# Order of ScalarE's work at two places of a fused attention and MLP kernel: a kv copy between two exponentials, and the parting of a tile ahead of W1's sums

## The reference

```
proj = x @ w_phi;  proj -= max|proj| over the 128 features
phi(x) = concat(exp(proj), exp(-proj))          # for q and for k
kv = phi(k)^T v;   z = sum over s of phi(k)
out = phi(q) kv / (phi(q) z + 1e-6)
```

```
block A:  u = x + Re(FFT over both axes of x);  un = layernorm(u);        u + relu(un @ w1a) @ w2a
block B:  un = layernorm(x) * g;                                          x + relu(un @ w1b) @ w2b
```

## Time and profile before

| | |
|---|---|
| median of 3 runs | 1027.41 us |
| the profiled execution's own time | 1027.07 us |
| its span, first to last instruction | 1025.0 us |
| PE busy | 1012.9 us, 99% |
| DVE, ACT, POOL busy | 64%, 58%, 36% |
| mean granted clock of PE | 0.998 |

### The profile page before, as it was taken

One profiled execution on the slowest core, in us unless ns is written; L12 is line 12 of the kernel. 1 busy time (PEld: TensorE's weight loads), 2 busy tenths in 40 slices (PEclk: granted clock), 3 DMA queues, 4 the chain that ended last, 5 costly groups with the idle time before them and its releaser, 6 DMA issues.

```text
span 1025.0 us, 17118 instructions
## 1 busy us (share of the span) xinstructions
PE 1012.9 (99%) x6028; PEld 936.4 (91%) x6028; DVE 657.5 (64%) x1156; ACT 591.8 (58%) x1036; POOL 368.5 (36%) x364
## 2 busy tenths in 40 slices
PE   7999999999999999999999999999999999999998
PEld 7999999999988998999989989989989989899897
DVE  5676776889966649556585556755568455674443
ACT  6766566686565555555556566566565566634341
POOL 5632442435144335134342234431353332721210
PEclk9999999999999999999999999999999999999999
DMA  6233122120252322322222322323315223233202
GB/s 160 66 80 91 39 68 70 36 48 12 79 132 74 98 72 64 102 83 72 73 82 84 103 64 73 101 62 94 95 50 155 83 72 103 62 123 83 62 1 62
DMA packets 101314, 80.32 MB, mean 78 GB/s; under 512 B 56944, under 2 KB 81776, under 8 KB 101232
## 3 DMA queue, kind: packets, MB, share of 16 engines
q1 hardware_dynamic: 100992, 78.91, 27.5%
q10 hardware_dynamic: 240, 0.33, 0.1%
HBM read 66.10 MB, written 4.72 MB: 69 GB/s over the span
## 4 chain that ended last, share of the span: by engine, by line
PE 92%; ACT 2%; DVE 2%; POOL 1%; DMA 1%; issue 1%; SPq 1%; DVEq 0%; ACTq 0%; POOLq 0%
PE bank L1185 37%; PE bank L1162 33%; PE bank L406 6%; PE bank L419 5%; PE bank L364 4%; PE bank L389 3%; PE bank L660 2%; PE bank L680 1%; PE bank L358 1%; PE bank L424 1%; DMA rawqk<-qkT 1%; DMA xT_high_halves<-xn 0%; ACT feat_q L503 0%; DVE xall L547 0%; PE bank L1123 0%
## 5 line engine op out<-in xcount | busy, mean ns | idle before, releaser
L1185 PE MATMUL bank<-w2op,hid 128*128 128x512 f32 x1728 | 426.8, 392 | 0.0
L1185 PEld LDWEIGHTS bank<-w2op,hid 128*128 128x128 f32 x1728 | 321.9, 188 | 57.0 <-issue 0.3
L1162 PE MATMUL bank<-x_T,w1op 128*128 128x384 f32 x1152 | 210.3, 338 | 1.9 <-ACT part_a L1428 1.9
L1162 PEld LDWEIGHTS bank<-x_T,w1op 128*128 128x128 f32 x1152 | 203.2, 189 | 6.0 <-issue 2.3
L1162 PE MATMUL bank<-x_B,w1op 128*128 128x384 f32 x864 | 173.5, 336 | 0.0
L1162 PEld LDWEIGHTS bank<-x_B,w1op 128*128 128x128 f32 x864 | 154.3, 188 | 11.2
L1357 POOL TENSOR_TENSOR w_sums<-st_w 128x256 f32<-128x256 f32 x48 | 49.3, 1027 | 226.6 <-DVE w1op L1393 222.7
L1473 DVE SCALAR_TENSOR_TENSOR hid<-part_s,hid 128x384 fp32r<-128x384 f32 x141 | 98.1, 722 | 37.3 <-ACT hid L1469 37.1
L1414 DVE TENSOR_TENSOR w2op<-st_w,w2op 128x1024 fp32r<-128x1024 f32 x48 | 64.5, 1344 | 46.7 <-ACT w2op L1410 46.6
L1325 POOL TENSOR_TENSOR x_sums<-xraw 128x256 f32<-128x256 f32 x30 | 22.3, 768 | 200.4 <-ACT xraw L1277 125.2
L1469 ACT ACTIVATE hid<-part_s 128x384 fp32r<-128x384 f32 x141 | 73.4, 525 | 31.3 <-DVE part_s L1443 31.0
(11 more groups left out here) (181 smaller groups left out, 1612.7 us busy)
## 6 DMA issues: line engine op xcount, KB each, us to landing
st_w<-w1a SPq DMA_DIRECT2D x24, 512.0 KB, 3.4
st_w<-w2a SPq DMA_DIRECT2D x24, 512.0 KB, 3.8
st_w<-w1b SPq DMA_DIRECT2D x24, 512.0 KB, 3.4
st_w<-w2b SPq DMA_DIRECT2D x24, 512.0 KB, 3.7
v<-v SPq DMA_DIRECT2D x16, 256.0 KB, 3.1
out<-xall SPq DMA_DIRECT2D x16, 256.0 KB, 2.1
rawqk<-qkT SPq DMA_DIRECT2D x14, 288.0 KB, 4.0
rawqk<-qkT SPq DMA_DIRECT2D x14, 256.0 KB, 3.7
```

The lines of the kernel that those rows point to most:

```text
L1162: last = nc.tensor.matmul(dst, w1op[g % 2][:, a, W1OP.index(w), c, :], xop[x][:, b, c, :], start=name in ("M2", "M1", "M7") and k_ == 0, s ...
L1185: last = nc.tensor.matmul(acc[t0 + t][:, :], hid[name, g % 2][:, x, P * t:P * (t + 1)], w2op[g % 2][:, y, j, :], start=first and k_ == 0, ...
```

## The change

Two places change, both in the order of instructions; none is added or taken out.

At the first, ACT's list for pairs 0 and 1, the exponentials of q of pair 1 are issued one at a time, and the second kv copy of pair 0 goes between them. At the second, period 1 of the MLP, the parting of tile 0 of group 1 goes right behind W2's rounding, then the hidden blocks 22 and 21, and only then the high part of W1's sums of period 2, on ACT; on DVE the low parts of the hidden blocks 22 and 21 go ahead of the low part of W1's sums. All other periods keep their order.

```diff
-    def act_exp(act, g, which):
+    def act_exp(act, g, which, halves=(0, 1)):
...
-        for f, sc in ((0, 1.0), (1, -1.0)):
+        for f in halves:
             nc.scalar.activation(feat[which][:, :, FEAT * f:FEAT * (f + 1)], shift[which][:, :, :],
-                                 ACT.Exp, scale=sc).then_inc(exd[which], 1)
+                                 ACT.Exp, scale=(1.0, -1.0)[f]).then_inc(exd[which], 1)
...
             if g == 1:
                 act_std(act, 1)
                 act_w2_hi(act, 1)
+                act_halves(act, 1, 0)
+                act_hid(act, 1, "22")
+                act_hid(act, 1, "21")
             if n == FP_ - 1 and nxt:
                 act_x_hi(act, i + 1, 2)
                 act_x_hi(act, i + 1, 3)
             if g + 1 < NP:
                 act_w1_hi(act, g + 1, 3)
-            act_hid(act, g, "22")
-            act_hid(act, g, "21")
+            if g > 1:
+                act_hid(act, g, "22")
+                act_hid(act, g, "21")
             if n == 0 and nxt:
                 act_std(act, i + 1)
-            if g == 1:
-                act_halves(act, 1, 0)
-            elif next_tile(g) is not None:
+            if g > 1 and next_tile(g) is not None:
                 act_join(act, i + 1, next_tile(g))
             act_hid(act, g, "12")
...
                 dve_ln_rstd(dve, 1)
                 dve_xn(dve, 1, 0)
                 dve_w2_lo(dve, 1)
+                dve_hid_lo(dve, 1, "22")
+                dve_hid_lo(dve, 1, "21")
             if g + 1 < NP and late:
                 dve_w1_lo(dve, g + 1, 1)
                 dve_w1_lo(dve, g + 1, 2)
             if g + 1 < NP:
                 dve_w1_lo(dve, g + 1, 3)
-            dve_hid_lo(dve, g, "22")
-            dve_hid_lo(dve, g, "21")
+            if g > 1:
+                dve_hid_lo(dve, g, "22")
+                dve_hid_lo(dve, g, "21")
...
             act_q_copy_out(act, 0, 4)
-            act_exp(act, 1, "q")
+            act_exp(act, 1, "q", (0,))
             act_kv_copy(act, 0, 1)
+            act_exp(act, 1, "q", (1,))
             act_exp(act, 1, "k")
```

## The result

The changed kernel took **1023.44 us** in the median of 18 executions (1023.03 to 1024.63), the kernel before, run beside it, 1027.67 us (1023.52 to 1030.29). The ratio is 0.9963, 95% interval 0.9953 to 0.9974. The forecast was 1023.4 us, in a range of 1022.5 to 1025.2, with 0.88 for faster: value, range and direction held. The spread is the first thing that the prediction had not told: the kernel before scatters over 6.8 us, the changed one over 1.6. The experiments show that the forecast sum was right and its shares, taken over many executions, were not.

What follows compares the result with a forecast made beforehand. TensorE, busy 99%, bounds the kernel, so only its waits and clock could gain: 2.12 + 1.64 + 0.20 = 3.96 us off 1027.07 gives 1023.1; with 0.34 to the median, 1023.4 us, range 1022.5 to 1025.2.

Steps and rivals of the forecast that it cites:

- The sum: Whole kernel: 2.12 us from the part_a stall, 1.64 from the clock fall behind it, 0.20 from pair 0; 3.96 us.
- First place, geometry: Pair 0: PE's 0.82 us wait behind the second kv copy goes, 0.62 returns as a wait for qfT.
- give-back: Near 30 us: ACT's copy of transposed q, behind the rawqk load and split, takes back 0.62 of 0.82 us.
- First place, price: Pair 0: gain of 0.20 us, bounds 0 to 0.82, with no clock fall behind the kv wait.
- Rival A: Pair 0 keeps its whole 0.82 us because the rawqk load comes earlier: 4.58 us gained, 1022.8 us; chance 0.12.
- Second place, chain: Period 1: parting 1.51 us earlier, transposes issued 291.75 and 293.13, landing 295.5, PE restarting at 299.55 without the stall.
- covers: Period 1: work moved back still precedes its reader, 4.8 us for W1's sums, 0.8 for block 12's low part.
- Second place, price: Period 1: 2.12 us from PE's stall behind part_a plus 1.64 from the clock fall behind it.
- Rival B: Period 1: part of the stall stays, an instruction fetch meeting the transposes, 0.8 us stall, 1024.2 us; chance 0.15.
- Rival B's other half: Period 1: block 12's low part slow beside POOL's sums, M1 stalls 0.8 us, 1024.2 us; within the 0.15 chance.
- Rival C: The clock falls all the same behind a smaller wait: 2.32 us gained, 1025.1 us; chance 0.05.
- Rival D: Period 1: transposes meet the W loads and land late; 1027.9 us, or 1029.6 with a clock fall; chance 0.12.

Runs made afterwards that it cites:

- e3: The kernel before, run again with no edit, to see its spread; its profiled execution took 1029.01 us.
- e6: Changed kernel with ACT's round 1 copy of transposed q moved ahead of the split in pair 2's slot; median 0.77 us under the changed kernel's.
- e2: The kernel before with only the second place (period 1) edited; median 1025.79 us.
- e1: The kernel before with only the first place (pair 0) edited; mean 1.89 us less, ratio 0.9979.
- e9: Changed kernel with tile 0's parting moved from period 1 to behind W2's rounding of period 2; median 1.7 us above the kernel before's 1027.53.
- e5: Changed kernel with W1's sums again ahead of hidden blocks 22 and 21, on ACT and DVE; median 1024.19 us.
- e8: Changed kernel with pair 0's second kv copy behind both q exponentials and the first of k; median 1029.74 us.

## Why the prediction was right, and where it was not

**The sum** of 3.96 us met 3.4 to 4.2 (mean and median differences, in three sets): right. Between the two profiled executions it came term by term: 0.11 us from all that lies ahead of period 2 (297.71 less 297.60), 2.09 from the stall (4.16 less 2.07) and 1.61 from the 24 matmuls (5.97 less 4.36), 3.81 in all, against 0.20 + 2.12 + 1.64. But that was luck. The execution on which the sum rests is one of a scatter over 6.8 us, and it happened to lie 0.34 us from the median; the same working on an execution without the stall, or on one like e3's, would have given another sum. The median loses about as much, but in many of its executions at the other place.

**First place, geometry (what PE's waits give without the clock): right.** The 0.82 us wait went, and a wait for qfT behind the rawqk load came, 0.52 to 0.90 us in the six profiles that have this order. From the kv products to the transposes, the six take 8.92 to 9.31 us, where the kernel before takes 9.27, so 0.35 us at most is left; I had said 0.20. And e6 shows that the give-back is the copy's place behind the split.

**First place, price: wrong.** "The 0.82 us wait did not bring one, as the mean of 0.998 leaves room for no second" was true of one execution and was carried over to all. In e2 the clock fell behind this wait, in 6 of 12 by the mean clock. The term that I took at 0.20 us, with 0.82 as the upper bound, measured 1.89 us (0.94 to 2.84). Rival A, 0.82 us kept, had too small a price as well. The mistake is the bound: it left the clock out of this place although it had the clock as a term at the other.

**Second place, chain: right** to about 0.1 us at every step, issue, landing, join, part_a, restart. The covers held too: block 12's low part ended at 295.63 (forecast 295.7), POOL's sums began at 294.88 (294.8).

**Second place, price: too high as an average.** The 2.12 + 1.64 us were the price in an execution with a 4.4 us landing and a fall. Over many executions the edit alone gave 0.97 us (-0.30 to 2.27). In e1, with the old order here, half of the executions show no sign of the stall, and five of the six others kept the clock. An estimate from these counts comes near both measured shares: half (e2's count) of a 3.4 us fall and 0.2 us at the first place, 1.9 us; half of a 2.1 us stall and a twelfth of a 1.6 us fall at the second, 1.2 us.

**Rival B, the fetch.** I wrote that the instruction fetch "follows PE's code and moves by 0.2 us". It does not: the packet starts near 295.9 us in the kernel before, near 298.9 in the changed kernel and near 301.3 in e1, although e1 issues the same instructions on PE and its transposes at the same times as the kernel before. The thirteen profiles fall into two kinds. In three (the kernel before, e3, e9) the packet starts 0.9 to 1.3 us behind the issue of tile 0's second transpose, and the transpose lands after 4.4, 4.3 and 3.7 us. In the other ten it starts 5.8 us or more behind, and the transpose lands after 2.3 or 2.4. That fits the collision without an exception, but it was only seen together; no run took the fetch away, so the cause stays open, as does the reason why the packet moves. Rival B's other half, M1 waiting for block 12, appeared in e5 at 0.27 us.

**Rival C** did not come, in 39 executions of the changed kernel: the wait near 31 us, 0.52 to 0.82 us in its three profiles, never brought the clock down. **Rival D** did not come: the first transpose issued into the loads and took 3.0 us to land, the second 2.4.

The Trainium skill (DMA: Bandwidth & Descriptors, Queues, rings and completion order) has each DMA engine take a ring's descriptors in order; a first transpose 0.6 us later than usual and a second on time agree with it, but would also agree with transfers that share the engines in another way.

## What to carry to other kernels

One profiled execution is one of many. Where the executions of a kernel scatter over more than the gain at stake, look at how time and mean clock go together over many of them before you price a term, and let every wait of PE have an upper bound with a clock fall in it. An edit that takes away a wait of under a microsecond may be worth more than the wait. And what a late DMA holds up should stand behind, not in front of, what PE needs next in an in-order list.

## What the runs showed of the hardware that I had not expected

- A wait of 0.82 us was followed by the half clock in 6 of 12 and 3 of 12 executions, one of 1.87 us at the same place in 12 of 12. In the middle of dense matmuls one of about 2 us was followed by it in 1 of 6, one of 3.35 us (in the profiled execution) in 10 of 12. The counts are by mean clock and time. What else than its length decides is open; the first place lies in the program's first 25 us, with other waits of PE around it and short matmuls.
- The fall need not come at once: in e8 PE runs on at 24.64 us, its clock is 1.00 in 22 to 26 us and 0.74 in 26 to 28.
- The landing of the same DMA transpose, issued at the same 294.64 us, took 4.4 us in one profile and 2.3 in another, and one packet of the instruction queue moved by 5.4 us (295.9 to 301.3) between these two profiles, which have the same instructions on PE.
